# Linear attention and two feed-forward layers in one kernel: token groups of 512 in place of 384

## The reference, cut to what matters

```python
# 1: linear attention with decay, B, H, S, D = 4, 8, 768, 64
for t in range(S):
    state = gamma * state + einsum('bhd,bhe->bhde', k[:, :, t], v[:, :, t])
    y[:, :, t] = scale * einsum('bhd,bhde->bhe', q[:, :, t], state)
# 2: x is (3072, 512); w_a, w_b (512, 1536); w_out (1536, 512)
x = ((x @ w_a) * (x @ w_b)) @ w_out
# 3: one of 8 experts for each token
e_idx = argmax(x @ w_gate, axis=1)
gate_w = softmax(x @ w_gate)[e_idx];  eom = sigmoid(x @ w_output_gate)[e_idx]
out[token] = gate_w * eom * (relu(x @ w1[e_idx]) @ w2[e_idx])
```

## Time and profile before

| | us |
|---|---|
| three runs | 1051.03, 1052.42, 1057.27 (median 1052.42) |
| the profiled execution | 1050.76 |
| its span, first to last instruction | 1048.9 |
| TensorE busy in it | 1026.0 |
| first up matmul of group 0 | at 87.76 |
| end of the last group | at 700.33 |

### The profile page before, as it was taken

How to read it: one execution, slowest core, us unless ns; L and a number is a source line. 1 busy time by engine, 2 the same in 40 slices (tenths; PEclk the granted TensorE clock), 3 DMA queues, 4 the chain that set the end, 5 groups by cost and what they waited for, 6 DMA issues and landing times.

```text
span 1048.9 us, 18935 instructions
## 1 busy us (share of the span) xinstructions
PE 1026.0 (98%) x6334; PEld 920.8 (88%) x6335; DVE 571.3 (54%) x1347; ACT 293.4 (28%) x550; POOL 110.7 (11%) x108
## 2 busy tenths in 40 slices
PE   6999999999999999999999999999999999999997
PEld 5888999999999999999999999987788888888886
DVE  3445444765765756747747742557454536354542
ACT  2444332212112122122122121231343424243431
POOL 4770000000000000000000000000211111211111
PEclk9999999999999999999999999999999999999999
DMA  9997904214104204113223111110835333345311
GB/s 362 368 326 219 238 1 128 64 31 142 52 31 141 69 20 143 62 48 118 65 82 90 51 62 63 67 51 21 301 117 190 127 118 120 127 149 176 117 35 36
DMA packets 48056, 123.99 MB, mean 118 GB/s; under 512 B 5997, under 2 KB 12461, under 8 KB 47984
## 3 DMA queue, kind: packets, MB, share of 16 engines
q1 hardware_dynamic: 42928, 108.37, 31.2%
q0 software_dynamic: 4480, 13.90, 3.8%
q10 hardware_dynamic: 576, 0.79, 0.2%
HBM read 105.71 MB, written 18.12 MB: 118 GB/s over the span
## 4 chain that ended last, share of the span: by engine, by line
PE 94%; DMA 4%; DVE 1%; issue 1%; POOL 0%; ACT 0%; ACTq 0%; DVEq 0%; POOLq 0%
PE bank L1026 38%; PE bank L1044 19%; PE bank L1386 14%; PE bank L1363 13%; PE bank L1371 2%; PE bank L591 2%; DMA rows<-in_steps 2%; PE bank L542 1%; PE bank L648 1%; DMA xg<-x_dram,idx_gather 1%; PE bank L556 1%; DMA qdec_t<-in_consts 1%; PE bank L577 1%; PE bank L932 0%; POOL out L1314 0%
## 5 line engine op out<-in xcount | busy, mean ns | idle before, releaser
L1026 PE MATMUL bank<-x_hi,wab_hi 128*128 128x384 f32 x768 | 257.8, 336 | 0.0
L1026 PE MATMUL bank<-x_hi,wab_lo 128*128 128x384 f32 x768 | 257.7, 336 | 0.0
L1026 PE MATMUL bank<-x_lo,wab_hi 128*128 128x384 f32 x768 | 257.2, 335 | 0.0
L949 DVE SCALAR_TENSOR_TENSOR products<-y_sb,gate_row 128x512 f32<-128x512 f32 x288 | 180.9, 688 | 0.0
L962 DVE TENSOR_TENSOR g_sb<-bank,b_sb 128x384 f32<-128x384 f32 x96 | 53.5, 558 | 186.3 <-PE bank L1026 185.0
L1026 PEld LDWEIGHTS bank<-x_hi,wab_hi 128*128 128x128 f32 x768 | 144.3, 188 | 4.3 <-issue 0.4
L1026 PEld LDWEIGHTS bank<-x_lo,wab_hi 128*128 128x128 f32 x768 | 144.2, 188 | 3.7
L1026 PEld LDWEIGHTS bank<-x_hi,wab_lo 128*128 128x128 f32 x768 | 144.1, 188 | 0.0
L1363 PE MATMUL bank<-w,xe_hi 128*128 (+1 forms) x432 | 136.2, 397 | 1.2 <-DVE xe_lo L657 1.1
L1044 PE MATMUL bank<-wo_hi,g_lo 128*128 128x512 f32 x288 | 114.3, 397 | 0.0
L1044 PE MATMUL bank<-wo_lo,g_hi 128*128 128x512 f32 x288 | 114.2, 396 | 0.0
(11 more groups left out here) (166 smaller groups left out, 1143.6 us busy)
## 6 DMA issues: line engine op xcount, KB each, us to landing
raw<-in_w SPq DMA_DIRECT2D x64, 512.0 KB, 5.0
gate_row<-xT_dram SPq DMA_DIRECT2D x96, 256.0 KB, 3.2
rows<-in_steps SPq DMA_DIRECT2D x20, 768.0 KB, 7.7
rows<-in_steps SPq DMA_DIRECT2D x24, 256.0 KB, 7.3
wab_raw<-in_weights SPq DMA_DIRECT2D x24, 256.0 KB, 8.0
x_dram<-y_sb SPq DMA_DIRECT2D x8, 768.0 KB, 4.2
xT_dram<-x_all SPq DMA_DIRECT2D x6, 768.0 KB, 11.4
x_raw<-xT_dram SPq DMA_DIRECT2D x6, 768.0 KB, 6.8
```

The source lines that it names most:

```text
L949: nc.vector.scalar_tensor_tensor(products[n % 2], y_sb[:, t], 1.0, gate_row[e % GATE_SLOTS], ALU.mult, ALU.mult, accum_out=L3[:, t, e:e + ...
L1026: ins = nc.tensor.matmul(bank[to][:, 0:GT], wab(w, f, j), x[s][:, k, :], start=(k == 0 and m == 0), stop=(k == KD - 1 and m == 2))
```

## The change

The groups have 512 tokens: 6 groups of 4 tiles. An up matmul has 512 columns and fills a PSUM bank. The down products need four banks (4 to 7), so the up products turn through banks 0, 1 and 2 (`b_bank`, `a_bank`), and bank 3 is `spare` for what bank 7 was used for. The second half of up(f) waits for `b_read` of f-1. To make room, `x_raw` lies in the buffer of the low part of x of the same parity; its load (four DMAs, one per tile, in pieces of 128 values) waits until the group before the last one has been multiplied (`a_done`). `b_sb`, `g_sb` and `g_lo` are one buffer, and there is one `products` buffer: each dot waits for the one before it. `DOTS_AT` is spread anew for 64 dots, the ranking comes a step later, SP's order of stores and weight loads in the first group is changed, and some tables and expert buffers are moved; the tile table now lies where `y_sb` was and waits for its store. The core of the diff:

```diff
-GT = 384
+GT = 512
...
-DOTS_AT = (0, 6, 6, 3, 6, 3, 5, 6, 6, 6, 1, 0)
+DOTS_AT = (4, 7, 7, 3, 7, 6, 6, 6, 7, 7, 4, 0)
...
+    x1_hi = place("x1_hi", (P, KD, GT), F32R)
+    x1_raw, x1_lo = place("x1_raw", (P, KD, GT), where=at[0]), place("x1_lo", (P, KD, GT), F32R)
...
     b_sb = place("b_sb", (P, 2, GT))
-    g_sb_at = at[0]
-    g_sb = place("g_sb", (P, 2, GT))
+    g_sb = place("g_sb", (P, 2, GT), where=gb_at)
+    g_lo = place("g_lo", (P, 2, GT), F32R, where=gb_at)
     g_hi = place("g_hi", (P, 2, GT), F32R)
...
-    products = [place(f"products{n}", (P, DM), where=(product_at, after_x + DM * 4)[n]) for n in range(2)]
+    products = place("products", (P, DM))
...
+    spare = bank[3]
+
+    def b_bank(f):
+        return bank[2 * f % 3]
+
+    def a_bank(f):
+        return bank[(2 * f + 1) % 3]
...
-    def load_x(sp, g):
-        sp.dma_start(x_raw.rearrange("p i k t -> p (i k t)"),
-                     x_groups[bass.ds(g, 1)].rearrange("a p c -> (a p) c")).then_inc(x_raw_in, 16)
+    def load_x(sp, g, s):
+        frm = x_groups[bass.ds(g, 1)].rearrange("a p (i k t) -> (a p) i k t", i=TG, k=KD)
+        for i in range(TG):
+            sp.dma_start(x_raw[s][:, :, i * P:(i + 1) * P], frm[:, i]).then_inc(x_raw_in, 16)
...
-                sp.wait_ge(x_lo_done, KD * (g + 1))
                 load_gate_rows(sp, g, range(GATE_SLOTS))
-                load_x(sp, g + 1)
+                sp.wait_ge(a_done, KF * g)
+                load_x(sp, g + 1, 1 - s)
...
                 act.wait_ge(b_done, n + 1)
-                act.wait_ge(g_done, n - 1 + 2)
-                nc.scalar.copy(b_sb[:, f % 2], bank[2 * (f % 2) + 1][:, 0:GT]).then_inc(b_read, 1)
+                act.wait_ge(down_done, n - 1 + 2)
+                nc.scalar.copy(b_sb[:, f % 2], b_bank(f)).then_inc(b_read, 1)
                 act.wait_ge(g_done, n + 1 + 2)
-                act.wait_ge(down_done, n - 1 + 2)
...
-            if n > 1:
-                dve.wait_ge(dots_done, DOTS * g + n - 1)
-            nc.vector.scalar_tensor_tensor(products[n % 2], y_sb[:, t], 1.0, gate_row[e % GATE_SLOTS], ALU.mult, ALU.mult,
+            if n > 0:
+                dve.wait_ge(dots_done, DOTS * g + n)
+            nc.vector.scalar_tensor_tensor(products, y_sb[:, t], 1.0, gate_row[e % GATE_SLOTS], ALU.mult, ALU.mult,
...
-            for which, to, done in ((1, 2 * (f % 2) + 1, b_done), (0, 2 * (f % 2), a_done)):
+            for which, to, done in ((1, b_bank(f), b_done), (0, a_bank(f), a_done)):
+                if which == 0 and n > 0:
+                    pe.wait_ge(b_read, n)
...
-                        ins = nc.tensor.matmul(bank[to][:, 0:GT], wab(w, f, j), x[s][:, k, :],
+                        ins = nc.tensor.matmul(to, wab(w, f, j), x[s][:, k, :],
...
+        dve.wait_ge(x_out, 16 * GROUPS)
         link(v.tensor_copy(pair_i, e_end[:, NE - 1:NE]))
```

More of the change, by code:

```diff
@@ L168, in build @@
     at[0] = after_w
-    x1_hi, x1_lo = (place(f"x1_{n}", (P, KD, GT), F32R) for n in ("hi", "lo"))
+    x1_hi = place("x1_hi", (P, KD, GT), F32R)
+    x1_raw, x1_lo = place("x1_raw", (P, KD, GT), where=at[0]), place("x1_lo", (P, KD, GT), F32R)
     x0_at = at[0]
-    x0_hi, x0_lo = (place(f"x0_{n}", (P, KD, GT), F32R) for n in ("hi", "lo"))
-    x_hi, x_lo = (x0_hi, x1_hi), (x0_lo, x1_lo)
+    x0_hi = place("x0_hi", (P, KD, GT), F32R)
+    x0_raw, x0_lo = place("x0_raw", (P, KD, GT), where=at[0]), place("x0_lo", (P, KD, GT), F32R)
+    x_hi, x_lo, x_raw = (x0_hi, x1_hi), (x0_lo, x1_lo), (x0_raw, x1_raw)
     small_at = at[0]
@@ L230, in build @@
     xg_first = (xg[0], place("xg_first1", (P, DM), where=yT_sb_at + 2 * DM * 4))
[L231 to L243, removed]
+    xe_lo = place("xe_lo", (P, 2, KD, P), F32R, where=yT_sb_at + 3 * DM * 4)
+    at[0] = common
+    part_last = place("part_last", (P, GT))
+    yT_last = place("yT_last", (P, KD, GT))
     at[0] = common
@@ L407, in sp_weights @@
         stored(2)
-        stored(3)
         load_wab(sp, 2)
@@ L783, in on_pe, with apart @@
         return g - (GROUPS - 2)
+    def apart(g):
+        return bank[7] if isinstance(g, int) and g == GROUPS - 1 else spare
     def pe_yT(pe, g, t):
@@ L791, in pe_yT @@
         for k in range(KD):
-            ins = nc.tensor.transpose(bank[7][:, k * P:(k + 1) * P], y_sb[:, t, k * P:(k + 1) * P], ident)
+            ins = nc.tensor.transpose(spare[:, k * P:(k + 1) * P], y_sb[:, t, k * P:(k + 1) * P], ident)
         ins.then_inc(yT_done, 1)
@@ L800, in pe_partial @@
             strip = slice(k * (P // KD), (k + 1) * (P // KD))
-            ins = nc.tensor.matmul(bank[7][strip, 0:GT], gates_pad[:, k, :], yT[:, k, :], start=True, stop=True)
+            ins = nc.tensor.matmul(apart(g)[strip], gates_pad[:, k, :], yT[:, k, :], start=True, stop=True)
         ins.then_inc(part_done, 1)
@@ L806, in pe_logits @@
         for t in range(TG):
-            ins = nc.tensor.matmul(bank[7][:, t * 2 * NE:(t + 1) * 2 * NE], part[:, t * P:(t + 1) * P], sel, start=True, stop=True)
+            ins = nc.tensor.matmul(apart(g)[:, t * 2 * NE:(t + 1) * 2 * NE], part[:, t * P:(t + 1) * P], sel, start=True, stop=True)
         ins.then_inc(logit_done, TG)
@@ L826, in pe_rank @@
             pe.wait_ge(logit_read, TG * (on_pe(g) + 1))
-        to = bank[7][:, 0:TG * NE]
+        to = apart(g)[:, 0:TG * NE]
         nc.tensor.matmul(to, tri, g_key8.rearrange("p t e -> p (t e)"), start=True, stop=False)
@@ L929, in pe_first_slots @@
         pe.wait_ge(first_hot_done, 1)
-        nc.tensor.matmul(bank[7][:, FIRST_COUNT:FIRST_COUNT + 1], ones_t, seen[:, TG, 0:1], start=True, stop=True)
+        nc.tensor.matmul(spare[:, FIRST_COUNT:FIRST_COUNT + 1], ones_t, seen[:, TG, 0:1], start=True, stop=True)
         for t in range(TILES - TG):
-            ins = nc.tensor.matmul(bank[7][:, 0:FIRST], off_hot[:, t, :], hot_first[:, t, :],
+            ins = nc.tensor.matmul(spare[:, 0:FIRST], off_hot[:, t, :], hot_first[:, t, :],
                                    start=(t == 0), stop=(t == TILES - TG - 1))
@@ L1059, in group @@
                         pe_logits(pe, g - 1)
-                if not first and f == AT_SCALE:
+                if not first and f == (AT_SCALE if last else DOT_RANK - 1):
                     pe_rank(pe, g - 1)
```

97 lines of the change are left out of this document (50 added, 47 removed).

## The result

The changed kernel takes 1040.78 us (median of four runs, 1039.93 to 1041.68), the kernel before 1051.72 on the same chips (1050.69 to 1057.27): a ratio of 0.9885, 95% interval 0.9849 to 0.9921. It is 10.9 us or 1.15% faster; forecast were 4.8 us, with a range whose low end was 1042.5. The profiled execution took 1039.93 us, its span is 1038.1 for 1048.9.

What follows compares the result with a forecast made beforehand. TensorE, busy 98% of the span, was taken as the bound; -7.5 - 0.8 + 0 + 1.8 + 0.8 + 0.9 = -4.8 us, from a usual 1051.4 to 1046.6 us. The range was 1042.5 to 1052.3.

Steps and rivals of the forecast that it cites:

- Up products: Feed-forward up matmuls: 2304 of 384 columns become 1728 of 512, 24 taking 5.47 us; -7.5 us.
- Rival B: Up matmuls run at the down matmuls' 231 ns, fixed part not saved: -2.0 instead of -7.5, 1052.1 us; chance 0.13.
- Down products: Feed-forward down matmuls keep their number (864) and width, 12 in four banks instead of 9 in three: 0.
- Ranking: Small ranking matmuls in the middle groups: two groups fewer have them at 0.4 us each, -0.8 us.
- VectorE and ScalarE: Middle groups: their work, at most 7.9 us on VectorE, fits the 8.25 us step, dots 0.72 us apart; cost 0.
- rival C: VectorE becomes the bound through slower dots in four middle groups; at 1.2 us a dot +40, 1086 us; chance 0.03.
- rival D: Turning through three banks makes the granted clock fall once per group: +10 us, 1056.8 us; chance 0.03.
- Attention: Attention stage: GpSimd's wider x_lo splits (1.30 us each) delay the k decay and the last v rows; +1.8 us.
- rival A: Attention stage hides the longer splits: cheap split, or DMA queue never runs dry; 1044.8 us, chance 0.20.
- Last group: Last feed-forward group: one more tile to transpose, wider partial logits and logits, one small matmul fewer; +0.8 us.
- Routing tail: Routing behind the last group: one more tile of transposes and a longer VectorE chain; +0.9 us, bounds 0.4 and 1.7.

Runs made afterwards that it cites:

- e5: Changed kernel with 256 columns in up and down matmuls (down of step 0 keeps 512), half the work left out; 24 up matmuls took 2.87 us.
- e1: Changed kernel with each up matmul taking only 384 of its 512 columns, down matmuls, buffers and banks unchanged; 967.5 us as a whole.

## Why the forecast was wrong

The direction was right and the size was not: -4.8 forecast, -10.9 measured, and the time is below the range. Faster by over 1%, which came, had been given 0.06. Point by point:

- **Up products** (-7.5 forecast): -9.8. The reason was right, a part of each matmul that isn't columns and doesn't grow: 13.3 ns at 384 and at 512, and 576 matmuls less are 7.7 us. Mis-sized was the row: "5.47, the row that has both the width and the twelve in one bank". It has transposes with 128 columns on either side (L1371 and L648 of the kernel before), and so is a disturbed row itself: 5.44 is what the width takes. And 4.18 of before was a disturbed row as well, some 0.02 of it. Rival B (231 ns) fell; its 5.55 gives -1.7, not the -2.0 of the prediction, which changes nothing here. The 2.5 ns that the Trainium skill ("TensorE: Matmul & The Clock Gate", "Wait — 56ns, not 53.3ns?") has as the fixed part of a matmul aren't what stands here: 13 ns at 256, 384 and 512 columns, with a weight load before each matmul.
- **Down products** (they "keep their number", so 0): -4.0. This is the step that failed. I had 231 and 228 ns for the same 512 columns in two stages on the table, and put the difference down to the bank, which changes every third matmul. Now the bank changes every third matmul as before and the distance is 226.7. The neighbours' width was nearly all of the difference; the runs with 384 beside 512 columns in the new buffers, and with 384 alone in the old ones, show it. Together with its share in the up products the equal width is worth 6.3 us, and with the 7.7 of the fixed part 14.0, for 13.8 measured.
- **Ranking** (-0.8): -0.8.
- **VectorE and ScalarE** (0): 0. The dots stand 0.73 to 0.74 us apart (0.72 taken), as the timeline of VectorE shows:

```profile
294.91 0.69 DVE L962 SCALAR_TENSOR_TENSOR products<-y_sb,gate_row 128x512 f32<-128x512 f32 x1 [1.62 <-DMA gate_row<-xT_dram]
...
295.64 0.69 DVE L962 SCALAR_TENSOR_TENSOR products<-y_sb,gate_row 128x512 f32<-128x512 f32 x1
...
296.38 0.69 DVE L962 SCALAR_TENSOR_TENSOR products<-y_sb,gate_row 128x512 f32<-128x512 f32 x1
```

  (the read of the accumulator stands between them). The first dot of a group waits 1.6 us for its gate row, VectorE is busy for 66.8 of 98.4 us, and PE waits for it nowhere in the middle groups: rival C fell. The x loads, now in pieces of 512 bytes, came in time.
- **The clock** (rival D): 1.00 in the middle groups with three banks in turn; the one dip behind the small matmuls of the last group is there as before. What the Trainium skill (the same page, "A second HAM failure mode: psum-queue depth-cycling") tells of cycling through banks did not show in these runs: in rows of matmuls with 512 columns the granted clock stayed. The page puts its case down to short idle times of PE between groups of matmuls; here PE was busy for 98.38 of the 98.38 us, so its rule was not put to the test.
- **Attention** (+1.8): +1.3 in one profile of the changed kernel, +1.8 in the other. GpSimd's split took 1.24 us a piece (4.98 for four, 1.30 taken). In the second profile PE waited 1.49 us for the decayed k and stood 1.2 us later there than before (61.62 for 60.41, 1.5 forecast), and the v rows landed at 81.4, as forecast. Of rival A the cheap split fell; that the stage as a whole pays for the wait is likely and not shown, since the starts scatter from 87.7 to 92.5 us. That both profiles lie near the forecast is in part luck: the prediction had no term for the pauses or the clock behind them.
- **Last group** (+0.8): +1.3. **Routing tail** (+0.9): +1.2. Both have short matmuls (transposes with 128 columns, logits with 16) between long ones, one set more than before, and the bounds of the tail (0.4 to 1.7) held; 16 transposes of the last group take 1.75 us where 12 took 1.31:

```profile
691.09 1.75 PE bank L1100 x16
...
694.21 1.05 PE bank L810 x8
...
696.85 0.81 PE bank L816 x8
```

## What to carry to other kernels

Before pricing a matmul by a row elsewhere in the trace, look at what stands on either side of it: here the same 512 columns cost 226.7 ns among their like and 231 in the mean (224 to 236) beside 384, so making two loops' widths equal paid almost as much (6.3 us) as issuing a quarter fewer of the up matmuls (7.7 us). When two rows with the same shape differ, take the difference apart position by position before giving it a cause. And a longer operation on an engine that is off the path has to be checked against the slack at each place where it stands: wider pieces on GpSimd (1.24 us each) became a wait of 1.49 us on TensorE in the attention stage, and moving them behind the work that others wait for took a few lines. And where an engine stands still with no releaser, look at where in its program it does so and at the instruction queues, before a theory of the change is built on it.

## What the hardware showed that was not expected

- In a row of weight load and matmul pairs the distance is N/2.4 GHz + 13 ns at 256, 384 and 512 columns at the full clock (120, 173.3, 226.7), and 112 ns at 128, more than the 67 that this would give. At half clock it is N/1.2 GHz with nothing on top at 256 and 512 columns (213 in e5, 427 in e1).
- Matmuls of 384 and of 512 columns in turn: after the change to 384 five of the first six are slow (26 ns in all), after the change to 512 eight of the first nine (41 ns). The pattern is the same within a nanosecond or so in each step and in two kernels with other buffers and banks, and it follows some pauses between matmuls of one width too. With 448 beside 512 columns the narrower ones go round in fives and never settle.
- With 128 columns in all matmuls the granted clock fell to 0.57 in the mean from 300 to 400 us, so 1.2 GHz most of the time, although the profile shows PE busy for 98.05 of these 100 us. A busy share near 1 is no sign that the clock stays.
- On PE pauses of 0.1 to 2.9 us came without any wait that the profile names, in the stage in which the DMA engines are at 0.7 of their time and more, at six fixed places 123 to 125 matmuls apart, and each ended 1.2 to 1.9 us behind the end of a 16 KB packet of an instruction queue.
- Behind pauses of 2.05, 2.60 and 2.92 us the granted clock fell to half, behind those of 1.80 and 2.06 it stayed.
